# Attention and two expert layers on one core: the last V load ahead of a weight load, two weight splits on VectorE, casts and ranks one duo apart

## Time and profile before

| what | value |
|---|---|
| median of 3 runs | 1228.59 us (1223.77 to 1229.87) |
| the profiled execution, its own time | 1218.38 us |
| its span, first to last instruction | 1216.7 us |
| TensorE busy | 1175.0 us (97%) |
| VectorE, ScalarE, GpSimd busy | 701.4 us, 436.5 us, 802.2 us |
| mean granted TensorE clock | 0.987 of full speed |
| TensorE's share of the chain that ended last | 93% |
| HBM traffic | 149 GB/s over the span |

### The profile page before, as it was taken

How to read it: one execution, slowest core, us unless ns; L and a number is a source line. 1 busy time by engine, 2 the same in 40 slices (tenths; PEclk the granted TensorE clock), 3 DMA queues, 4 the chain that set the end, 5 groups by cost and what they waited for, 6 DMA issues and landing times.

```text
span 1216.7 us, 19284 instructions
## 1 busy us (share of the span) xinstructions
PE 1175.0 (97%) x6446; PEld 1023.4 (84%) x6447; DVE 701.4 (58%) x1589; ACT 436.5 (36%) x920; POOL 802.2 (66%) x541
## 2 busy tenths in 40 slices
PE   8999869899999999999999999999999999999996
PEld 6777747688888888999889999999999999999995
DVE  6777737232222247666666666666666666666664
ACT  6777731111211143333333333333333333333330
POOL 6657764856666766658758776678568676666662
PEclk8999979999999999999999999999999999999998
DMA  8997955888888803212111132122211221111111
GB/s 292 321 309 237 330 212 195 321 289 315 319 319 319 304 26 123 79 55 77 68 70 70 69 122 96 69 87 66 83 69 70 87 98 60 60 65 66 71 35 52
DMA packets 47853, 181.75 MB, mean 149 GB/s; under 512 B 10016, under 2 KB 16160, under 8 KB 32032
## 3 DMA queue, kind: packets, MB, share of 16 engines
q1 hardware_dynamic: 28880, 111.95, 26.2%
q0 software_dynamic: 9536, 56.64, 13.1%
q10 hardware_dynamic: 9360, 12.17, 3.0%
HBM read 161.45 MB, written 19.36 MB: 149 GB/s over the span
## 4 chain that ended last, share of the span: by engine, by line
PE 93%; DVE 2%; DMA 2%; issue 2%; ACT 1%; POOLq 0%; ACTq 0%; POOL 0%; DVEq 0%
PE ps L1853 33%; PE ps L1796 28%; PE ps L1710 9%; PE ps L1694 9%; PE ps L1623 3%; PE ps L1607 2%; PE ps L1639 2%; PE ps L1595 1%; PE ps L1721 1%; DMA x_rows<-x_by_expert 1%; PE ps L1596 1%; PE ps L1655 1%; ACT scores_probs L884 0%; DMA qk_raw<-q_k_turned 0%; PE ps L1749 0%
## 5 line engine op out<-in xcount | busy, mean ns | idle before, releaser
L1552 DVE SCALAR_TENSOR_TENSOR out_sums<-ps,share_token,out_sums 128x512 f32<-128x512 f32 x270 | 202.5, 750 | 134.5 <-PE ps L1853 133.3
L1853 PE MATMUL ps<-w_hi,h_hi 128*128 128x512 f32 x576 | 226.7, 394 | 0.0
L1853 PE MATMUL ps<-w_hi,h_lo 128*128 128x512 f32 x576 | 226.3, 393 | 0.0
L1796 PE MATMUL ps<-x_hi,w_hi 128*128 128x384 f32 x672 | 224.8, 334 | 1.2 <-DVE h_lo L1536 1.2
L1853 PE MATMUL ps<-w_lo,h_hi 128*128 128x512 f32 x576 | 225.9, 392 | 0.0
L1796 PE MATMUL ps<-x_lo,w_hi 128*128 128x384 f32 x672 | 224.9, 335 | 0.0
L1796 PE MATMUL ps<-x_hi,w_lo 128*128 128x384 f32 x672 | 224.8, 334 | 0.0
L766 POOL TENSOR_TENSOR w_lo<-w_raw,w_hi 128x1024 fp32r<-128x1024 f32 x48 | 115.2, 2401 | 160.4 <-ACT w_hi L1031 160.3
L646 POOL TENSOR_TENSOR w_split<-w_raw,w_split 128x2048 fp32r<-128x2048 f32 x31 | 142.1, 4588 | 69.2 <-DMA w_split<-weights 42.2
L1058 ACT ACTIVATE h_hi<-ps 128x384 fp32r<-128x384 f32 x192 | 90.4, 493 | 206.8 <-DVE ps L1521 152.7
L761 POOL TENSOR_TENSOR w_lo<-w_raw,w_hi 128x1024 fp32r<-128x1024 f32 x48 | 116.0, 2416 | 55.1 <-ACT w_hi L1042 55.0
(11 more groups left out here) (231 smaller groups left out, 1865.7 us busy)
## 6 DMA issues: line engine op xcount, KB each, us to landing
w_raw<-weights SPq DMA_DIRECT2D x80, 1024.0 KB, 4.6
w_split<-weights POOLq DMA_DIRECT2D x32, 1024.0 KB, 8.1
qk_split<-q_k_turned POOLq DMA_DIRECT2D x9, 1152.0 KB, 9.9
qk_raw<-q_k_turned SPq DMA_DIRECT2D x14, 576.0 KB, 5.3
v<-v_tiles SPq DMA_DIRECT2D x16, 320.0 KB, 4.6
y_sorted<-y ACTq DMA_DIRECT2D x20, 256.0 KB, 3.9
x_rows<-x_by_expert ACTq DMA_DIRECT2D x19, 256.0 KB, 5.5
x_by_expert<-zeros SPq DMA_DIRECT2D x16, 260.0 KB, 9.2
```

What stands on the lines that cost most here:

```text
L1552: v.scalar_tensor_tensor(out=a_, in0=ps[:, 4 + t % 3, :], scalar=share_, in1=a_, op0=ALU.mult, op1=ALU.add).then_inc(acc_done, 1)
L1796: last = mm(ps[:, bank, 0:HALF_T], wt[:, w, c * P:(c + 1) * P], xt[:, c, x, :], start=(k == 0), stop=(k == 3 * KC - 1))
L1853: last = mm(ps[:, 4 + t % 3, :], ht[:, f, t * P:(t + 1) * P], wt[:, f, :], start=(k == 0), stop=(k == n - 1))
```

## The change

- SyncE: `load_raw(2, first)` moves out of the last step of the loop to right behind the loop, so it stands behind the last `load_v` and ahead of the early rows.
- GpSimd: split 2 and the wait for `scores_ready` ahead of it go. VectorE makes it in `split_down(2)`, between `xt_low(1)` and `h_low(0)`; `split_down(3)` behind `h_low(0)` is the split that was there.
- ScalarE: the two casts of k are made in the last two duos of a pair, one in each, with their waits.
- VectorE: `miss`, `jumps` and `reaches` come 9, 10 and 11 duos behind the third batch, each in its own duo, where all three came 13 behind.
- TensorE and VectorE: `rank` comes 6 in place of 5 duos behind a batch, and `read_ranks` 7 in place of 6.
- TensorE: `WARM_SECOND` = 5 more products that nobody reads, ahead of the second head's wait in duo 0.

```diff
--- before.py
+++ after.py
@@ -345,6 +345,7 @@
         RAW_AFTER = NP - 3
         TURN_EARLY = DUOS + 2
         WARM_FIRST = 5
+        WARM_SECOND = 5
         PIECES = [(1, 0), (1, 1), (0, 0), (0, 1)]
         SPLIT_AT = [PIECES[0:2], PIECES[2:4]]
         ZEROS_MADE = 7
@@ -481,9 +482,6 @@
                     for i in range(EARLY):
                         sp.dma_start(xs_dram[e * CAP + i * P:e * CAP + (i + 1) * P, :], zeros[:]).then_inc(zeroed, 16)
 
-                if n == NP - 1:
-                    load_raw(2, first)
-
                 sp.wait_ge(pv_done, (n - 1) * QT)
                 load_v(n, n % 2)
                 if n == RAW_AFTER:
@@ -493,6 +491,7 @@
                     apart(sp)
                 if RAW_AFTER <= n < RAW_AFTER + 2:
                     load_raw(n - RAW_AFTER, first)
+            load_raw(2, first)
 
             sp.wait_ge(scattered, 16 * QT * (B - 1))
             for i in range(EARLY):
@@ -662,8 +661,6 @@
             pool.wait_ge(reach_made, 1)
             split(0, 0, 0, TOP1_ORDER[0])
             split(0, 0, 1, TOP1_ORDER[1])
-            pool.wait_ge(scores_ready, DUOS - QT)
-            split(0, 0, 2, TOP1_ORDER[2])
             pool.wait_ge(logits_summed, B)
             for i in range(2):
                 load_hi(1, second, i, TOP1_ORDER[i])
@@ -908,11 +905,11 @@
                     act.wait_ge(shifted, b + 1)
                     a.activation(exp_l[:, :, 0:E1], shift_l[:], ACT.Exp).then_inc(exps, 1)
                 n = j // QT + 2
-                if j % QT == QT - 1 and ACT_CASTS <= n < NP:
+                if j % QT >= QT - 2 and ACT_CASTS <= n < NP:
                     act.wait_ge(scores_ready, (n - 2) * QT)
                     act.wait_ge(qk_in[n % 2], raw_loads_of(n))
-                    for h in range(2):
-                        a.copy(qkh[:, hi_buffer(n), 1, h], qk_sb[:, n % 2, 1, h]).then_inc(k_cast, 1)
+                    h = j % QT - (QT - 2)
+                    a.copy(qkh[:, hi_buffer(n), 1, h], qk_sb[:, n % 2, 1, h]).then_inc(k_cast, 1)
                 if j == TURN_EARLY + 1:
                     x_high(0)
             act.wait_ge(shifted, B)
@@ -1352,13 +1349,13 @@
                 v.tensor_copy(reach[:, 0, :], tt[:, 5, 0:nt + EARLY]).then_inc(reach_made, 1)
 
             CHOICE = {13: (most_rows, choose, exchange), 14: (name_places, name_first), 18: (exchange_counts, exchange_rows)}
-            AHEAD = {13: (miss, jumps, reaches)}
+            AHEAD = {9: (miss,), 10: (jumps,), 11: (reaches,)}
             ROUTE = {3: (shift, pick, mark), 5: (gate_sum, gate_share), 7: (count,), 8: (add_ranks, put)}
 
             for j in range(DUOS + LAGS):
                 if j < DUOS:
                     mask_scores(2 * j)
-                for b in batch_due(j, 6):
+                for b in batch_due(j, 7):
                     read_ranks(b)
                 if j < DUOS:
                     mask_scores(2 * j + 1)
@@ -1405,13 +1402,17 @@
             put(last)
             relu_high(0)
             xt_low(1)
+
+            def split_down(i):
+                dve.wait_ge(split_done, i)
+                dve.wait_ge(hi_in[i], 16)
+                dve.wait_ge(raw_in[i % 2], 16 * 2)
+                v.tensor_tensor(Wl[0][:, TOP1_ORDER[i], :], raw[:, i % 2, :],
+                                Wh[0][:, TOP1_ORDER[i], :].bitcast(F32), ALU.subtract).then_inc(split_done, 1)
+
+            split_down(2)
             h_low(0)
-
-            dve.wait_ge(split_done, CHUNKS - 1)
-            dve.wait_ge(hi_in[CHUNKS - 1], 16)
-            dve.wait_ge(raw_in[1], 16 * 2)
-            v.tensor_tensor(Wl[0][:, TOP1_ORDER[CHUNKS - 1], :], raw[:, 1, :],
-                            Wh[0][:, TOP1_ORDER[CHUNKS - 1], :].bitcast(F32), ALU.subtract).then_inc(split_done, 1)
+            split_down(3)
 
             first_id = past8[0:1]
             full = sel[:].rearrange("p t e -> p (t e)")[:, 0:E1 * (nt + EARLY)].rearrange("p (e t) -> p e t", e=E1)
@@ -1589,6 +1590,9 @@
                     if j == 0 and hd == 0:
                         pe.wait_ge(first_split, 1)
                     elif t == 0:
+                        if n == 0:
+                            for i in range(WARM_SECOND):
+                                mm(ps[:, 4, 0:2 * P], ident[:], mask[:], start=True, stop=True)
                         pe.wait_ge(qk_lo, n + 1)
                     o = ps[0:m, j % BANKS, hd * 2 * P:hd * 2 * P + w]
                     lhs = qkh[:, hi_buffer(n), 0, hd, t * P:t * P + m]
@@ -1666,7 +1670,7 @@
                     pv(j - PV_LAG)
                 if 0 <= j - BACK_LAG < DUOS:
                     back(j - BACK_LAG)
-                for b in batch_due(j, 5):
+                for b in batch_due(j, 6):
                     pe.wait_ge(consts, CONSTS)
                     rank(b)
                 if j == TURN_EARLY:
```

## The result

Median 1211.48 us (20 runs, 1206.88 to 1223.82) against 1226.49 us (20 runs, 1219.78 to 1234.80) of the kernel before on the same chip. The ratio is 0.9894 (0.9869 to 0.9919), faster by 1.06%; applied to the 1228.59 us of the start it gives 1215.6. The forecast, 1218.1 us, is a ratio of 0.9915. The profiled execution took 1210.77 us, its span is 1209.2; the forecast for it was 1207.9.

The account below looks back on a forecast made before the run. It took TensorE's last chain, started late by the stall for V, as the bound. Tail -6.7, casts -1.1, ranks -1.2 and start -1.5 gave -10.5 us, so a median of 1218.1 us; range about 1208 to 1224.

Parts of the forecast that it names:

- The V stall: Last pair's probs times V: TensorE's 11.75 us idle time goes, as V is issued near 150 us and lands before 161.7.
- The row wait: At turn_rows(0) TensorE waits 4.9 us for early rows landing at 171.1 us; 10.5 us saved there.
- TensorE drains at full clock ... it arrives at turn_rows(0) at 166.2: Last pairs' drain up to turn_rows(0): 4.5 us at full clock in place of 8.1.
- The clock falls again: Behind the row wait TensorE's clock most likely halves, making the first half of up(0) 2.8 us longer.
- The first rival: Clock holds at the row wait: tail -10.2 us in place of -6.7, total -14.0, 1214.6 us; chance 0.15.
- the rule of a free-running monitor: At the row wait: the activity monitor doesn't restart with the kernel, so the clock may fall in one execution, hold in another.
- VectorE's second split: Split 2 on VectorE ahead of h_low(0) delays what stands behind it: +0.7 us, bounds 0 and 3.3.
- the third rival: VectorE's two splits hold up the last scatter, third tile's rows come late: total -4.5 us, 1224.1 us; chance 0.12.
- Casts and ranks: In attention, k casts in two duos shorten probs_t waits, -1.1 us; ranks a duo later remove waits for x, -1.2.
- The start: Five extra products cost a certain 1.0 us but hold the clock from 12 to 19 us: -1.5 us, bounds +1.0 and -1.8.
- Miss, jumps and reaches: Made earlier and apart, they let split 0 start right after the scatter; otherwise 0 us, bounds 0 to +0.3.

Follow-up runs that it names:

- raw_back: The changed kernel with load_raw(2) put back ahead of the last V: 1216.85 us, ratio 0.9950 to the kernel before.
- rows_first: The changed kernel with load_raw(2) moved on behind the loads of the early rows: 1208.94 us, ratio 0.9881 to the kernel before.
- no_lock: The changed kernel with two small VectorE copies written as tensor_reduce over one element: 1205.56 us, ratio 0.9850 to the kernel before.
- nl_split_pool: no_lock with split 2 back on GpSimd behind split 1: 1208.31 us, ratio 0.9857 to the kernel before.
- best: rows_first plus no_lock's reductions, without the extra start products, counts exchanged a duo later, row numbers written by the reduction: 1197.51 us, ratio 0.9796.
- best_hi: best with the last cast load of a weight chunk issued behind the third batch's scatter instead of ahead: 1203.30 us, ratio 0.9829.
- nl_casts: no_lock with the two k casts of a pair back together in its last duo: 1209.47 us, ratio 0.9862 to the kernel before.
- raw_ahead: raw_only with miss, jumps and reaches 9, 10 and 11 duos behind the third batch: 1213.14 us, ratio 0.9911 to the kernel before.
- raw_only: The kernel before with only load_raw(2) moved behind SyncE's loop: 1220.36 us, ratio 0.9961.

## Why the prediction was right, and where its steps were not

**The V stall: right.** V issued at 153.04 us (forecast: near 150), no idle time before probs times V, and the stall returns when the load goes back (raw_back).

**The row wait: right in place, wrong in size.** 1.57 us in place of 4.9, and turn_rows(0) still came 9.6 us earlier against duo 70 (7.9 + 1.7), where I had 10.5. The drain was late, far more than the rows: TensorE was done 15.9 us behind the copy of duo 70, where I had 11.7, and the rows came 0.8 us late. "TensorE drains at full clock ... it arrives at turn_rows(0) at 166.2" is the step that failed. It left out VectorE's stop of 3.02 us, which cost 2.19 us of TensorE's time and the full clock from 164.4 to 167.8. The rows landed 5.4 us behind the issue of load_raw(2), where I had 5.5. With rows_first the wait is none, as the same step says.

**The clock falls again: right, but not for the reason given.** 0.66 at 174 us and 0.63 at 180, with the first half of up(0) 2.28 us longer (forecast 2.8). My reason was that 4.9 us of idle time is more than the 3.9 after which the clock fell before; it fell behind a wait of 1.57 us, 2.6 us after TensorE had gone idle, and that it did so is luck. The first rival, that it holds, is out for this execution; rows_first shows the case without a wait. By the rule of a free-running monitor that stood beside that rival (the Trainium skill, TensorE: Matmul & The Clock Gate, "What's actually happening") the loss may differ from run to run. With one profiled execution of each kernel no run here shows that. Between kernels waits of like length did differ: behind its row wait of 1.81 us no_lock lost the clock for 3.4 us (0.61 at 172 us), the changed kernel for 6.8, and in nl_split_pool the clock held through a wait of 2.20 us at duo 72.

**VectorE's second split: +0.7 was right where it stood.** The third tile's x_low came 12.07 us behind the first product of down(0), in place of 11.39, and TensorE had lost 0.8 us by turn_rows of the fourth tile. First the kernel before, then the changed one:

```profile
198.40 0.61 PE L1710 MATMUL ps<-w_split,h_t_hi 128*128 128x512 f32 x2
209.79 0.69 DVE L1205 TENSOR_TENSOR x_t_lo<-ps,x_t_hi 128x512 fp32r<-128x512 f32 x1 [0.42 <-ACT x_t_hi L947]
227.20 0.66 PE L1655 MATMUL ps<-ident,x_rows 128*128 128x128 f32 x4 [0.63 <-DMA x_rows<-x_by_expert]
229.12 0.73 PE L1710 MATMUL ps<-w_split,h_t_hi 128*128 x2 [1.27 <-issue]
```
```profile
192.45 0.62 PE L1714 MATMUL ps<-w_split,h_t_hi 128*128 128x512 f32 x2
204.52 0.67 DVE L1202 TENSOR_TENSOR x_t_lo<-ps,x_t_hi 128x512 fp32r<-128x512 f32 x1
```

What the term left out are the last two rows of the kernel before, waits of 0.63 us for rows and of 1.27 us for something the profile doesn't name. The changed kernel has neither, and with them 2.1 us came back. That is not the split's work as far as can be told: from down(0) to down of the third tile the fourteen profiles take 27.4 to 32.4 us, those with one split 27.4 to 30.8, those with two 27.5 to 32.4. The two scatter issues were each stretched, as in the third rival, to 2.49 and 3.10 us, but the last one ended before the table (197.01 us), so nothing waited for it:

```profile
187.35 2.49 POOL L634 DMA_INDIRECT x_by_expert<-x,token_place  x1 [0.30 <-issue]
190.15 3.10 POOL L634 DMA_INDIRECT x_by_expert<-x,token_place  x1 [0.30 <-issue]
186.72 2.28 DVE L1410 TENSOR_TENSOR w_split<-w_raw,w_split 128x2048 fp32r<-128x2048 f32 x1
...
197.01 0.17 DVE L1439 CAST tile_x_row<-table_by_tile 1x27 int32<-1x27 f32 x1
...
204.44 0.16 DVE L1473 TENSOR_SCALAR expert_down_end<-table_by_expert 1x8 int32<-1x8 f32 x1
```

x_low of the third tile stands right behind expert_down_end, as forecast.

**Casts and ranks: right, the shares somewhat off.** Between duos 25 and 65 the changed kernel won 2.5 us (76.7 against 79.2), where the two terms say 2.3. Single stretches of five duos tell them apart over all profiles. Duos 50 to 55 and 60 to 65 took 10.1 and 9.9 us in all four kernels with the casts paired, and 9.4 to 9.6 and 9.3 us with them apart (in the second stretch nl_split_pool, best and best_hi took 11.8 to 14.6 for other reasons). That is 1.1 us for the casts, my number, and perhaps 0.5 us more between duos 40 and 50 (nl_casts against no_lock), where the profiles scatter more. Duos 25 to 30, where the first ranks fall, took 10.0 us in the kernel before and 8.9 to 9.4 in the nine kernels with ranks a duo later and no catch there; with a catch they took 12.8 us in the three kernels with ranks early and 12.0 in nl_casts. So ranks carry 0.8 us there, under my 1.2, and no later stretch shows more clearly. What I did not see at all is the new wait for qk_raw. I had named a wait of ScalarE for VectorE's scores ahead of the earlier cast, and never asked when the cast's own input lands.

**The start: mis-sized.** 1.0 us ahead at duo 10 in this execution where I had 1.5; over the kernels, nothing. The step that failed is "five 128x256 f32 products took 4.63 us at 1.2 GHz, so 2.2 us at 2.4", with "That price is certain" behind it: in half of the kernels with them they took 4 us, since the clock was not up yet.

**Miss, jumps and reaches: as forecast.** The split follows the scatter by 1.09 us, and raw_ahead shows that these three alone do it.

**What was missing** is the 5.1 us between duos 10 and 25, a term that the sum doesn't have. I had looked at each moved VectorE operation for its busy time and its readers, and never at what GpSimd does at the same moment. Without it duo 70 would be 3.4 us ahead (5.1 - 1.7), and my terms say 3.8. So the profiled execution came 2.9 us later than forecast. That the total is near all the same is in part good fortune. The profile of the kernel before lay under the whole range of its twenty runs (1218.38 against 1219.78 to 1234.80), so a usual run of it has losses that its profile doesn't show. My 10.5 us lie between the 7.6 of the profiles and the 13.0 of the ratio (0.0106 of 1228.59), and the range held, but the difference of the medians isn't the sum that I made.

**Open.** VectorE's stop at duo 72, 2.3 to 3.1 us with no engine's work before it, is in the changed kernel and in all eight of the first two sets, not in the kernel before and in none of the four of the third, among them raw_ahead, which differs from raw_only in three small operations. No edit of these runs goes with it; the set does, and with the set the chip, but no kernel was profiled in two sets, so neither is shown. Nor was each group of the changed kernel's runs profiled. Its nine slower runs have a mean granted clock of 0.984 to 0.989, its eleven faster ones 0.990 to 0.995, so the groups differ in time at the low clock; that catches and the wait for qk_raw make the difference rests on their size, 4 to 6 us each, and is not shown. The profiled run had a catch and is in the faster group all the same. And the cheapest cure of that wait, the k load ahead of the raw load or the cast behind the copy of probs_t, wasn't tried.

## What to carry to other kernels

When a load is moved in a queue, list what it now stands ahead of, and try both orders: here the V and the rows both wanted to be ahead of the same weight load, and the second order took the last wait away. Before a small operation is moved, look in the trace at what GpSimd runs at that time and at when its own input lands: a hold of 2 to 3 us in VectorE, or a wait as long in ScalarE, cost 4 to 6 us where TensorE's clock fell behind it, and little elsewhere. A reduction over one element in place of a copy was not held. To price an edit, choose two marks between which nothing else differs: a stretch that holds another low clock says nothing about the edit, as the split counted from up(0) showed. When a kernel's runs fall in two groups, compare the pace of like steps over several profiles before trusting one.
